# Reciprocal seed by exp of minus ln in block 0 of a fused attention, rational-FFN and gated-FFN kernel

## Chip, core and metric

One core of a Trainium2 chip. The metric is the device time of the kernel in microseconds (us). The engines are PE (TensorE, matmul), DVE (VectorE), ACT (ScalarE), POOL (GpSimd) and SP (SyncE, which issues DMAs here).

## What is computed

Three stages on 6016 tokens with 256 channels, all in 32-bit floats:

```python
qn = q / (norm(q, axis=1) + 1e-6); kn = k / (norm(k, axis=1) + 1e-6)
a = softmax(kn.T @ qn / tau)             # 256 x 256
x = v @ a                                # 6016 x 256
h = x @ w_in                             # 256 -> 2048
P = a0 + a1*h + a2*h**2 + a3*h**3
Q = 1.0 + abs(b0)*abs(h) + abs(b1)*h**2
y = (P / (Q + 1e-6)) @ w_out             # 2048 -> 256
gate = sigmoid(y @ w_gate); val = y @ w_val          # 256 -> 1536
out = (gate * val) @ w_out2              # 1536 -> 256
```

The kernel forms M = a @ w_in once, and then h = v @ M.

## The kernel before

**Tiling.** Channels lie on partitions, and the tokens are cut into 16 blocks of 376. The 2048 columns of the hidden layer are 16 tiles of 128, taken in 8 pairs. One pair of a block is a slot; a slot's tensors are 128x752 (two tiles of 376 tokens). Pairs are counted through: pair 8 is the first of block 1. Matmul operands are held as a high and a low half (hi, lo), and a product is three matmuls (`product3`, lines 721 to 723). In block 0 the second product of the rational layer is different: `add_raw_y` (L816) multiplies the undivided 32-bit values.

**A slot for pair j.** PE's `hidden` writes h to `ps_h` (12 matmuls). ACT makes `poly` = -(a3*h + a2) (L489, Identity) and `ab` = |h| (L492, Abs), then `vb` = b1*|h| + b0 (L512). DVE makes the Horner steps `poly` = poly*h (L673) and (poly - a1)*h (L684); the second one frees `ps_h` for the next `hidden`. In slot 0 poly, ab and the Horner steps are done in two halves (L483, L485, L662 to L681). Then DVE makes `quad` = vb*ab (L700), which is Q - 1. ACT makes the `seed`, an estimate of 1/Q with a sign, by reading the bits of quad as an integer and taking Sigmoid of it with a scale (L528). One slot later DVE makes t = (quad + 1)*seed (L649) in place of quad, and `scaled` = (poly - a0)*seed in place of poly (L653). ACT makes `e2` by Square of t (L467), and DVE makes the first Newton step (t - 2)*poly (`newton`, L619) and then the quotient g = (e2 + c)*poly (`quotient`, L626), which takes in a second Newton step. `g` has the same memory as `seed`. Two slots after its own, pair j's g goes into PE's product to y.

**Buffers.** `poly`, `quad` and `seed` have two buffers each, `ab`, `vb` and `e2` one. So ACT's poly waits for `g_ready` of two pairs before, and `ab` for `quad_ready` of the pair before.

**Beside it in block 0.** In slots 0 to 5 PE also makes the rest of M, tiles 4 to 11 (`M_AT`, `m_tile` L734), and ACT and DVE split them (`split_m`, L405 and L556). `hidden` waits for `m_lo_ready` of the M tiles it reads: for j = 2, 4, 6 that is one split in the slot just before. In the last slot ACT and DVE split v for block 1 (`split_v`, L399 and L550). The 13 weight chunks of the later products are split by ACT (`weights_hi`, L393) and POOL (`weights_lo`, L365): ACT takes chunk 6 + j at the end of slot j, POOL chunk 5 + j after `h_read` of slot j. SP reloads a stage when POOL is done with its last chunk, and after all of them loads v for block 1. ACT's tables: Sqrt for the norms (L421), Exp for the softmax (L435, a preload), Sigmoid from slot 0 on (L515).

**Order.** Each engine's program is written out by hand and runs in order; the engines meet at semaphores. Block 0 and block 1 are straight code, blocks 2 to 15 a loop. From block 1 on, the gated layer of the block before runs between the pairs (`gate_and_value`, `add_o`), and it begins in block 1's slot 1, after y is split (L462, L631).

Of the kernel before, what the change touches and what calls it, by code (L numbers as in the profile page):

```python
# [17 lines left out]
P = 128  # L18


def attention_rational_gated_kernel(nc, q, k, v, tau, w_in, w_out1, coef_a, coef_b, w_gate, w_val, w_out2, out):
# [58 lines left out]
    with ExitStack() as ctx:  # L80
# [40 lines left out]
        def region(at, shape):  # L121
# [12 lines left out]
        e2 = region(8 * PW, (2, TB))  # L134
        v_in = region(9 * PW, (CC, TB))
# [24 lines left out]
        consts = sb("consts", [P, 6])  # L160
        c_seed, c_square = consts[:, 0:1], consts[:, 1:2]
        norm_guard, sum_guard = consts[:, 4:5], consts[:, 5:6]

# [31 lines left out]
            sem("horner1"), sem("horner2"), sem("quad_ready"), sem("seed_ready"))  # L195
        t_ready, scaled, newton1, e2_ready, g_ready = (
# [26 lines left out]
        for n in reversed(range(T2 // 4)):  # L223
            chunks.append((w2_v[:, 4 * n:4 * n + 4, :], w2_hi[:, 4 * n:4 * n + 4, :], w2_lo[:, 4 * n:4 * n + 4, :]))
        def staged(n):
            a = chunks[n][1].shape[1]
            return stage[STAGE_OF[n]].rearrange("p (a b) -> p a b", a=a)
# [117 lines left out]
        @block.gpsimd  # L345
        def _(pool):

            nc.gpsimd.memset(consts[:, 0:1], SEED_BIAS).then_inc(o_stored, 16)
            nc.gpsimd.memset(consts[:, 1:2], -RIPPLE_D)
            nc.gpsimd.memset(consts[:, 2:3], 0.0).then_inc(g_hi_ready, PAIRS)  # L350
            nc.gpsimd.memset(consts[:, 3:4], 0.0).then_inc(g_lo_ready, PAIRS)
            nc.gpsimd.memset(norm_guard, 1e-6)
            nc.gpsimd.memset(sum_guard, 1e-9)
# [13 lines left out]

            pool.wait_ge(v_lo_ready, 1)
            for n in range(EARLY_LO):
                weights_lo(n)  # L370

            def step(i, first, carry, head, tail):
                for j, now, late, old, gone, early, second, left in slots(i, first, carry, head, tail):
                    if isinstance(i, int) and i * PAIRS + j < len(chunks) - EARLY_LO:
                        pool.wait_ge(h_read, now + 1)
                        weights_lo(EARLY_LO + now)
                    if old is not None and not unsplit(old):
                        n = j % 2
                        pool.wait_ge(g_hi_ready, old + 1)
                        wait_count(pool, y_added, old + (-1))  # L380
                        nc.gpsimd.tensor_tensor(g_lo[n], g[n], as_f32(g_hi[n]),  # L381
                                                ALU.subtract).then_inc(g_lo_ready, 1)

            steps(pool, step)


        @block.scalar
        def _(act):
# [46 lines left out]
            nc.scalar.activation(consts[:, 3:4], consts[:, 1:2], ACT.Exp)  # L435
# [32 lines left out]

            def step(i, first, carry, head, tail):
                if splits_v(i, first):  # L470
                    split_v(i)
                for j, now, late, old, gone, early, second, left in slots(i, first, carry, head, tail):
                    n, o = j % 2, (j - 1) % 2
# [6 lines left out]
                    if is_block(i, 0) and j == 0:  # L480
                        for x, done, read in ((0, h_half, h_half_read), (1, h_done, h_read)):
                            act.wait_ge(done, 1)
                            nc.scalar.activation(poly[n][:, x, :], ps_h[:, x, :], ACT.Identity, scale=neg_a[:, 3:4],  # L483
                                                 bias=neg_a[:, 2:3])
                            nc.scalar.activation(ab[:, x, :], ps_h[:, x, :], ACT.Abs).then_inc(read, 1)  # L485
                    elif now is not None:
# [6 lines left out]
                    for n_m in M_AT[j] if is_block(i, 0) and j < len(M_AT) else ():  # L493
                        split_m(n_m)
                    if is_block(i, 0) and j == PAIRS - 1:
                        split_v(1)
# [17 lines left out]
                    if is_block(i, 0) and j == 0:  # L514
# [3 lines left out]
                    if (j > 0 or not tail) and late is not None:  # L518
                        square(o, late)
                    if early is not None:  # L520
                        split_gated(*early)
                    if now is not None:
                        act.wait_ge(quad_ready, now + 1)
                        if unsplit(now) or (is_block(i, 1) and j < 2):
                            wait_count(act, y_added, now + (-1))
# [14 lines left out]
                    if isinstance(i, int) and i * PAIRS + j < len(chunks) - EARLY_HI:  # L540
                        weights_hi(EARLY_HI + now)
# [5 lines left out]
        def _(dve):  # L547
# [90 lines left out]

            def step(i, first, carry, head, tail):
                if splits_v(i, first):  # L640
                    split_v(i)
                for j, now, late, old, gone, early, second, left in slots(i, first, carry, head, tail):
                    n, o = j % 2, (j - 1) % 2
                    if j == 0 and early is not None:
                        times_value(*early)
                    if late is not None:
# [13 lines left out]
                    if is_block(i, 0) and j == 0:  # L660
                        dve.wait_ge(h_half_read, 1)
                        nc.vector.tensor_tensor(poly[n][:, 0, :], poly[n][:, 0, :], ps_h[:, 0, :],  # L662
                                                ALU.mult).then_inc(half_horner1, 1)
                        dve.wait_ge(half_horner1, 1)
                        nc.vector.scalar_tensor_tensor(out=poly[n][:, 0, :], in0=poly[n][:, 0, :], scalar=neg_a[:, 1:2],
                                                       in1=ps_h[:, 0, :], op0=ALU.add, op1=ALU.mult)
                        dve.wait_ge(h_read, 1)
                        nc.vector.tensor_tensor(poly[n][:, 1, :], poly[n][:, 1, :], ps_h[:, 1, :],
                                                ALU.mult).then_inc(horner1, 1)
                    elif now is not None:  # L670
# [6 lines left out]
                    if is_block(i, 0) and j == 0:  # L677
                        dve.wait_ge(horner1, 1)
                        nc.vector.scalar_tensor_tensor(out=poly[n][:, 1, :], in0=poly[n][:, 1, :], scalar=neg_a[:, 1:2],
                                                       in1=ps_h[:, 1, :], op0=ALU.add,  # L680
                                                       op1=ALU.mult).then_inc(horner2, 1)  # L681
                    elif now is not None:
# [7 lines left out]
                    for n_m in M_AT[j] if is_block(i, 0) and j < len(M_AT) else ():  # L690
                        split_m(n_m)
                    if is_block(i, 0) and j == PAIRS - 1:
                        split_v(1)
# [7 lines left out]
                    if (j > 0 or not tail) and late is not None:  # L701
# [206 lines left out]
```

## Time and profile before

| what | value |
|---|---|
| median of 3 runs | 1222.3 us (1221.54 to 1222.46) |
| the profiled execution | 1222.51 us, span 1220.6 us |
| mean granted TensorE clock | 0.995 |
| PE busy | 1196.8 us (98%), 6770 matmuls |
| weight loads busy (PEld) | 1168.6 us (96%) |
| DVE busy | 1074.8 us (88%), 1379 instructions |
| ACT busy | 882.7 us (72%), 1267 instructions |
| POOL busy | 250.3 us (21%), 146 instructions |
| DMA | 33.81 MB, nearly all in the first 60 us |

The chain of work that ended last is 91% PE, 5% DVE, 2% ACT. Block 0's `hidden` products start at 53.19 (pair 0), 58.77, 68.18, 76.33, 83.98, 90.41, 98.34 and 104.76 us (pair 7), block 1's first two at 112.92 and 120.40 us. All times in rows are us from the span's start; an instruction's duration can overlap the next one's by about 0.1 us on ACT and DVE, so what counts in a sum is the distance from start to start.

### The profile page before, as it was taken

The numbers are of one execution on the slowest core, as the hardware profiler recorded it, in microseconds if no ns is written. First come the engines' busy times: TensorE is split into PE (matmuls) and PEld (weight loads), VectorE is DVE, ScalarE is ACT, GpSimd is POOL, SyncE is SP. The second block draws the span as 40 slices with busy tenths as digits, with TensorE's granted clock in tenths as the row PEclk, the third lists the DMA queues.
The fourth block names the chain that finished last, engine by engine and source line by source line (L and its number), as shares of the span: only waits on it lengthen the run. The fifth ranks groups of instructions, "written<-read, shape, count | busy, mean of one in ns | idle before, by whom it ended". The sixth has DMA issues, their size and how long they took to land.

```text
span 1220.6 us, 19533 instructions
## 1 busy us (share of the span) xinstructions
PE 1196.8 (98%) x6770; PEld 1168.6 (96%) x6770; DVE 1074.8 (88%) x1379; ACT 882.7 (72%) x1267; POOL 250.3 (21%) x146
## 2 busy tenths in 40 slices
PE   9977899999999999999999999999999999999998
PEld 8855799999999999999999999999999999999998
DVE  7689999998998999999898989989899999989843
ACT  6877778777786777778686777777677677868632
POOL 0432112211221221212121212122122121212110
PEclk9989999999999999999999999999999999999999
DMA  9810000000000000000000000000000000000000
GB/s 368 291 65 13 2 13 1 14 13 13 13 13 13 13 0 13 13 13 13 13 13 9 4 13 13 13 13 13 13 6 7 13 13 13 13 0 13 0 14 13
DMA packets 15866, 33.81 MB, mean 28 GB/s; under 512 B 1382, under 2 KB 6246, under 8 KB 15846
## 3 DMA queue, kind: packets, MB, share of 16 engines
q1 hardware_dynamic: 14982, 32.51, 7.5%
q10 hardware_dynamic: 864, 1.05, 0.3%
q8 instruction: 11, 0.18, 0.1%
q14 instruction: 9, 0.07, 0.0%
HBM read 27.39 MB, written 6.16 MB: 27 GB/s over the span
## 4 chain that ended last, share of the span: by engine, by line
PE 91%; DVE 5%; ACT 2%; issue 2%; DMA 0%; DVEq 0%; ACTq 0%
PE ps L721 17%; PE ps L723 17%; PE ps L722 17%; PE ps L804 7%; PE ps L805 7%; PE ps L806 6%; PE ps L838 5%; PE ps L840 5%; PE ps L839 5%; PE ps L763 4%; DVE work L673 1%; DVE work L700 1%; DVE work L619 1%; ACT work L489 1%; ACT work L492 1%
## 5 line engine op out<-in xcount | busy, mean ns | idle before, releaser
L381 POOL TENSOR_TENSOR g_parts<-work,g_parts 128x752 fp32r<-128x752 f32 x120 | 218.7, 1822 | 838.5 <-ACT g_parts L503 838.5
L489 ACT ACTIVATE work<-ps,neg_a 128x752 f32<-128x752 f32 x127 | 124.5, 981 | 149.8 <-PE ps L723 87.8
L721 PE MATMUL ps<-v_hi,m_hi 128*128 128x376 f32 x512 | 173.4, 339 | 14.2 <-DVE m_lo L556 7.7
L723 PE MATMUL ps<-v_hi,m_lo 128*128 128x376 f32 x512 | 172.8, 337 | 0.0
L722 PE MATMUL ps<-v_lo,m_hi 128*128 128x376 f32 x512 | 171.7, 335 | 0.0
L804 PE MATMUL ps<-g_parts,w_hi 128*128 128x376 f32 x480 | 160.5, 334 | 0.0
L805 PE MATMUL ps<-g_parts,w_hi 128*128 128x376 f32 x480 | 160.0, 333 | 0.0
L806 PE MATMUL ps<-g_parts,w_lo 128*128 128x376 f32 x480 | 159.4, 332 | 0.0
L673 DVE TENSOR_TENSOR work<-work,ps 128x752 f32<-128x752 f32 x127 | 118.5, 933 | 42.1 <-ACT work L492 40.3
L528 ACT ACTIVATE work<-work,consts 128x752 f32<-128x752 int32 x128 | 117.6, 919 | 51.9 <-DVE work L700 51.9
L614 DVE TENSOR_TENSOR work<-work,ps 128x376 f32<-128x376 f32 x192 | 103.6, 540 | 52.3 <-PE ps L723 39.4
L467 ACT ACTIVATE work<-work,consts 128x752 f32<-128x752 f32 x128 | 118.0, 922 | 24.7 <-DVE work L649 24.7
L626 DVE SCALAR_TENSOR_TENSOR work<-work 128x752 f32<-128x752 f32 x128 | 122.1, 954 | 14.2
L456 ACT ACTIVATE ys<-work 128x376 fp32r<-128x376 f32 x192 | 98.6, 514 | 45.0 <-PE ps L840 44.9
L721 PE MATMUL ps<-ys,wg_hi 128*128 128x376 f32 x384 | 128.0, 333 | 3.2 <-DVE ys L631 2.7
L512 ACT ACTIVATE work<-work,abs_b 128x752 f32<-128x752 f32 x128 | 130.4, 1019 | 0.2
L838 PE MATMUL ps<-ys,w_hi 128*128 128x376 f32 x384 | 129.1, 336 | 0.2 <-DVE ys L636 0.2
L684 DVE SCALAR_TENSOR_TENSOR work<-work,neg_a,ps 128x752 f32<-128x752 f32 x127 | 126.3, 995 | 3.0
L723 PE MATMUL ps<-ys,wv_lo 128*128 128x376 f32 x384 | 128.7, 335 | 0.0
L700 DVE TENSOR_TENSOR work<-work 128x752 f32<-128x752 f32 x128 | 128.5, 1004 | 0.1
L723 PE MATMUL ps<-ys,wg_lo 128*128 128x376 f32 x384 | 128.5, 335 | 0.0
L840 PE MATMUL ps<-ys,w_lo 128*128 128x376 f32 x384 | 128.5, 335 | 0.0
(113 smaller groups left out, 2846.3 us busy)
## 6 DMA issues: line engine op xcount, KB each, us to landing
work<-in_v SPq DMA_DIRECT2D x16, 376.0 KB, 3.0
out<-work SPq DMA_DIRECT2D x15, 376.0 KB, 2.3
kq<-in_k SPq DMA_DIRECT2D x9, 512.0 KB, 12.9
kq<-in_q SPq DMA_DIRECT2D x9, 512.0 KB, 15.1
before<-in_moe_w_out SPq DMA_DIRECT2D x5, 512.0 KB, 12.6
before<-in_moe_w_in SPq DMA_DIRECT2D x8, 256.0 KB, 7.3
before<-in_moe_w_gate SPq DMA_DIRECT2D x2, 512.0 KB, 9.5
before<-in_moe_w_val SPq DMA_DIRECT2D x2, 512.0 KB, 6.7
```

Source lines behind the costliest of these rows:

```text
L381: nc.gpsimd.tensor_tensor(g_lo[n], g[n], as_f32(g_hi[n]), ALU.subtract).then_inc(g_lo_ready, 1)
L489: nc.scalar.activation(poly[n], ps_h, ACT.Identity, scale=neg_a[:, 3:4], bias=neg_a[:, 2:3])
L673: nc.vector.tensor_tensor(poly[n], poly[n], ps_h, ALU.mult).then_inc(horner1, 1)
L700: nc.vector.tensor_tensor(quad[n], vb, ab, ALU.mult).then_inc(quad_ready, 1)
L721: nc.tensor.matmul(dst, l_hi, r_hi, start=(n == 0), stop=False)
L722: nc.tensor.matmul(dst, l_hi, r_lo, start=False, stop=False)
L723: last = nc.tensor.matmul(dst, l_lo, r_hi, start=False, stop=(n == len(parts) - 1))
L804: nc.tensor.matmul(acc_y[:, c, :], l_hi, r_hi, start=(j == 0 and x == 0), stop=False)
L805: nc.tensor.matmul(acc_y[:, c, :], l_hi, r_lo, start=False, stop=False)
L806: last = nc.tensor.matmul(acc_y[:, c, :], l_lo, r_hi, start=False, stop=(j == PAIRS - 1 and x == 1))
L838: nc.tensor.matmul(acc_o[:, c, :], l_hi, s_hi[n], start=(m == 0), stop=False)
L840: last = nc.tensor.matmul(acc_o[:, c, :], l_lo, s_hi[n], start=False, stop=(m == T2 - 1))
```

## The change

In block 0 alone, the seed is made as exp(-ln(quad + 1 + 1e-6)) by two ScalarE activations (Ln with the bias `q_one`, then Exp with scale -1), instead of the integer Sigmoid. The seed is positive now. The Square and the first Newton step are gone; the quotient is (t - 2)*poly. The region of `e2` serves as a third `poly` buffer (`first_poly`), so poly of pair j waits for the quotient of pair j - 3. The slot's instructions have an order of their own (`first_slot`): on ACT poly, ab, up to two M splits, v split, vb, a third M split, then the seed of pair j - 1 (in slot 0: of pair 0; in slot 1: none), then the weight copy; on DVE the Horner steps, the M splits, quad of pair j, then t and scaled of pair j - 1 (again pair 0 in slot 0, none in slot 1), and the quotient of pair j - 1. Pair 7's seed, t, scaled and quotient stand in block 1's slot 0, and the load of the Sigmoid table behind its Exp. The preload before the softmax is an Ln instead of an Exp. ACT's and POOL's weight chunks move one slot later from slot 1 on. `newton1` and `e2_ready` are raised by 8 at the start, since block 0 no longer counts them.

```diff
+        first_poly = poly + [e2]
...
+            nc.gpsimd.memset(q_one, Q_ONE)
...
-                    if isinstance(i, int) and i * PAIRS + j < len(chunks) - EARLY_LO:
+                    if is_block(i, 0) and j != 1 or is_block(i, 1) and j == 0:
                         pool.wait_ge(h_read, now + 1)
-                        weights_lo(EARLY_LO + now)
+                        weights_lo(EARLY_LO + max(now - 1, 0))
...
-            nc.scalar.activation(consts[:, 3:4], consts[:, 1:2], ACT.Exp)
+            nc.scalar.activation(consts[:, 3:4], consts[:, 0:1], ACT.Ln)
...
+            def first_seed(pair):
+
+                act.wait_ge(quad_ready, pair + 1)
+                wait_count(act, y_added, pair - 1)
+                nc.scalar.activation(seed[pair % 2], quad[pair % 2], ACT.Ln, bias=q_one).then_inc(logs, 1)
+                act.wait_ge(logs, pair + 1)
+                nc.scalar.activation(seed[pair % 2], seed[pair % 2], ACT.Exp, scale=-1.0).then_inc(seed_ready, 1)
...
+                    act.wait_ge(h_done, j + 1)
+                    wait_count(act, g_ready, j - 2)
+                    nc.scalar.activation(p, ps_h, ACT.Identity, scale=neg_a[:, 3:4], bias=neg_a[:, 2:3])
+                    act.wait_ge(quad_ready, j)
+                    nc.scalar.activation(ab, ps_h, ACT.Abs).then_inc(h_read, 1)
...
+                if j != 1:
+                    first_seed(max(j - 1, 0))
+                if j > 0:
+                    weights_hi(EARLY_HI + j - 1)
...
-                    if is_block(i, 0) and j == 0:
+                    if is_block(i, 1) and j == 0:
+                        first_seed(PAIRS - 1)
                         nc.scalar.activation(consts[:, 2:3], consts[:, 1:2], ACT.Sigmoid)
...
+            def first_seeded(pair):
+
+                n, p = pair % 2, first_poly[pair % 3]
+                dve.wait_ge(seed_ready, pair + 1)
+                nc.vector.scalar_tensor_tensor(out=quad[n], in0=quad[n], scalar=Q_ONE, in1=seed[n],
+                                               op0=ALU.add, op1=ALU.mult).then_inc(t_ready, 1)
+                dve.wait_ge(horner2, pair + 1)
+                nc.vector.scalar_tensor_tensor(out=p, in0=p, scalar=neg_a[:, 0:1], in1=seed[n],
+                                               op0=ALU.add, op1=ALU.mult).then_inc(scaled, 1)
+
+            def first_quotient(pair):
+
+                dve.wait_ge(t_ready, pair + 1)
+                dve.wait_ge(scaled, pair + 1)
+                nc.vector.scalar_tensor_tensor(out=g[pair % 2], in0=quad[pair % 2], scalar=-2.0,
+                                               in1=first_poly[pair % 3], op0=ALU.add,
+                                               op1=ALU.mult).then_inc(g_ready, 1)
...
+                first_quad(j)
+                for n_m in tiles[2:]:
+                    split_m(n_m)
+                if j != 1:
+                    first_seeded(max(j - 1, 0))
+                if j > 0:
+                    first_quotient(j - 1)
```

## Rows read from the trace of the kernel before

**Rows 1.** Stretches: window, then each engine's busy us, PE clock, DMA share.
```profile
80.00:90.00 10.00, 9.09 (x33) 5.72 (x32) 9.76 (x12) 8.65 (x12) 3.95 (x2) 1.00 0.28 93
...
180.00:190.00 10.00, 10.00 (x60) 10.00 (x59) 8.89 (x11) 5.92 (x8) 1.82 (x1) 1.00 0.12 39
```

**Rows 2.** Waits of PE, whole span: us in total, times, longest us.
```profile
PE ps L721 <- DVE m_lo L556: 7.7, 3, 5.4
...
PE ps L721 <- DVE v_lo L550: 2.2, 1, 2.2
```

**Rows 3.** Timeline of DVE, slot 4: start us, us, instruction, [idle before <- releaser].
```profile
88.38 0.94 DVE L673 TENSOR_TENSOR work<-work,ps 128x752 f32<-128x752 f32 x1
89.35 1.00 DVE L684 SCALAR_TENSOR_TENSOR work<-work,neg_a,ps 128x752 f32<-128x752 f32 x1
90.27 0.75 DVE L556 SCALAR_TENSOR_TENSOR m_lo<-ps,small,m_hi 128x512 fp32r<-128x512 f32 x1
90.93 0.93 DVE L700 TENSOR_TENSOR work<-work 128x752 f32<-128x752 f32 x1
91.78 0.94 DVE L619 SCALAR_TENSOR_TENSOR work<-work 128x752 f32<-128x752 f32 x1
92.82 0.94 DVE L626 SCALAR_TENSOR_TENSOR work<-work 128x752 f32<-128x752 f32 x1
93.68 0.93 DVE L649 SCALAR_TENSOR_TENSOR work<-work 128x752 f32<-128x752 f32 x1
94.53 0.99 DVE L653 SCALAR_TENSOR_TENSOR work<-work,neg_a 128x752 f32<-128x752 f32 x1
```

**Rows 4.** Timeline of ACT, slot 4.
```profile
86.68 0.98 ACT L489 ACTIVATE work<-ps,neg_a 128x752 f32<-128x752 f32 x1
87.56 0.79 ACT L492 ACTIVATE work<-ps 128x752 f32<-128x752 f32 x1
...
88.81 1.02 ACT L512 ACTIVATE work<-work,abs_b 128x752 f32<-128x752 f32 x1
...
91.89 0.93 ACT L528 ACTIVATE work<-work,consts 128x752 f32<-128x752 int32 x1 [1.26 <-DVE work L700]
```

**Rows 5.** Timeline of PE, slot 4: first hidden matmul, M tile, raw y, next hidden.
```profile
83.98 0.41 PE L721 MATMUL ps<-v_hi,m_hi 128*128 128x376 f32 x1 [0.91 <-DVE m_lo L556]
...
86.11 1.88 PE L734 MATMUL ps<-before 128*128 128x512 f32 x4
87.83 2.69 PE L816 MATMUL ps<-work,before 128*128 128x376 f32 x8
90.41 0.44 PE L721 MATMUL ps<-v_hi,m_hi 128*128 128x376 f32 x1
```

**Rows 6.** Timeline of ACT, slot 0: vb, table load, seed.
```profile
59.55 1.00 ACT L512 ACTIVATE work<-work,abs_b 128x752 f32<-128x752 f32 x1
60.57 1.28 ACT L515 ACT_TABLE_LOAD   x1
...
61.97 0.91 ACT L528 ACTIVATE work<-work,consts 128x752 f32<-128x752 int32 x1
```

**Rows 7.** Timeline of PE, slot 2: first hidden matmul and M tile.
```profile
68.18 0.65 PE L721 MATMUL ps<-v_hi,m_hi 128*128 128x376 f32 x1 [5.39 <-DVE m_lo L556]
...
72.08 2.17 PE L734 MATMUL ps<-before 128*128 128x512 f32 x4
```

**Rows 8.** A stretch in the gap before slot 2, columns as in rows 1.
```profile
66.00:68.00 2.00, 0.00 (x0) 0.00 (x0) 1.97 (x4) 1.66 (x2) 1.81 (x1) 0.50 0.00 0
```

**Rows 9.** Timeline of POOL and of DVE, slot 6.
```profile
102.78 2.37 POOL L365 TENSOR_TENSOR w_lo<-work,w_hi 128x1024 fp32r<-128x1024 f32 x1 [4.81 <-ACT work L492]
...
104.62 1.33 DVE L700 TENSOR_TENSOR work<-work 128x752 f32<-128x752 f32 x1
```

**Rows 10.** Timeline, block 1: t of pair 8 on DVE, first gate product on PE.
```profile
122.92 0.93 DVE L649 SCALAR_TENSOR_TENSOR work<-work 128x752 f32<-128x752 f32 x1
...
127.72 0.44 PE L721 MATMUL ps<-ys,wg_hi 128*128 128x376 f32 x1 [1.86 <-DVE ys L631]
```

More of the change, by code:

```diff
@@ L351, in _ @@
             nc.gpsimd.memset(consts[:, 3:4], 0.0).then_inc(g_lo_ready, PAIRS)
-            nc.gpsimd.memset(norm_guard, 1e-6)
-            nc.gpsimd.memset(sum_guard, 1e-9)
+            nc.gpsimd.memset(norm_guard, 1e-6).then_inc(newton1, PAIRS)
+            nc.gpsimd.memset(sum_guard, 1e-9).then_inc(e2_ready, PAIRS)
+            nc.gpsimd.memset(q_one, Q_ONE)
             nc.gpsimd.memset(ones[:], 1.0).then_inc(consts_ready, 1)
@@ L467, in square, with first_slot @@
                 nc.scalar.activation(e2, quad[o], ACT.Square, scale=RIPPLE_D, bias=c_square).then_inc(e2_ready, 1)
+            def first_seed(pair):
[4 more added lines that the diff above has]
+                nc.scalar.activation(seed[pair % 2], seed[pair % 2], ACT.Exp, scale=-1.0).then_inc(seed_ready, 1)
+            def first_slot(j):
+                p = first_poly[j % 3]
+                if j == 0:
+                    for x, done, read in ((0, h_half, h_half_read), (1, h_done, h_read)):
+                        act.wait_ge(done, 1)
+                        nc.scalar.activation(p[:, x, :], ps_h[:, x, :], ACT.Identity, scale=neg_a[:, 3:4],
+                                             bias=neg_a[:, 2:3])
+                        nc.scalar.activation(ab[:, x, :], ps_h[:, x, :], ACT.Abs).then_inc(read, 1)
+                else:
+                    act.wait_ge(h_done, j + 1)
[3 more added lines that the diff above has]
+                    nc.scalar.activation(ab, ps_h, ACT.Abs).then_inc(h_read, 1)
+                tiles = M_AT[j] if j < len(M_AT) else ()
+                for n_m in tiles[:2]:
+                    split_m(n_m)
+                if j == PAIRS - 1:
+                    split_v(1)
+                act.wait_ge(h_read, j + 1)
+                nc.scalar.activation(vb, ab, ACT.Identity, scale=abs_b[:, 1:2],
+                                     bias=abs_b[:, 0:1]).then_inc(vb_ready, 1)
+                for n_m in tiles[2:]:
+                    split_m(n_m)
+                if j != 1:
+                    first_seed(max(j - 1, 0))
+                if j > 0:
+                    weights_hi(EARLY_HI + j - 1)
             def step(i, first, carry, head, tail):
@@ L479, in step @@
                         square(o, late)
-                    if is_block(i, 0) and j == 0:
[L481 to L486, printed above, removed]
+                    if now is not None:
                         act.wait_ge(h_done, now + 1)
@@ L517, in step @@
                         split_y(i)
-                    if (j > 0 or not tail) and late is not None:
+                    if (j > 0 or not tail) and late is not None and not unsplit(late):
                         square(o, late)
@@ L523, in step @@
                         act.wait_ge(quad_ready, now + 1)
-                        if unsplit(now) or (is_block(i, 1) and j < 2):
-                            wait_count(act, y_added, now + (-1))
+                        if is_block(i, 1) and j < 2:
+                            act.wait_ge(y_added, now - 1)
                         else:
@@ L637, in split_gated, with first_quad @@
                                         ALU.subtract).then_inc(s_lo_ready, 1)
+            def first_quad(pair):
+                dve.wait_ge(vb_ready, pair + 1)
+                nc.vector.tensor_tensor(quad[pair % 2], vb, ab, ALU.mult).then_inc(quad_ready, 1)
+            def first_seeded(pair):
[6 more added lines that the diff above has]
+                                               op0=ALU.add, op1=ALU.mult).then_inc(scaled, 1)
@@ L645, in step @@
                         times_value(*early)
-                    if late is not None:
+                    if late is not None and not unsplit(late):
                         dve.wait_ge(seed_ready, late + 1)
@@ L659, in step @@
                         quotient(o, late)
[L660 to L670, printed above, removed]
+                    if now is not None:
                         dve.wait_ge(h_read, now + 1)
@@ L676, in step @@
                         times_value(*early)
[L677 to L682, printed above, removed]
+                    if now is not None:
                         dve.wait_ge(horner1, now + 1)
@@ L689, in step @@
                         split_gated(*left)
[L690 to L693, printed above, removed]
                     if j == y_split_at(i) and head:
@@ L700, in step @@
                         nc.vector.tensor_tensor(quad[n], vb, ab, ALU.mult).then_inc(quad_ready, 1)
-                    if (j > 0 or not tail) and late is not None:
+                    if late is not None and unsplit(late):
+                        first_seeded(late)
+                        first_quotient(late)
+                    elif (j > 0 or not tail) and late is not None:
                         newton(o, late)
```

44 lines of the change are left out of this document (36 added, 8 removed).

## Prediction

> **What bounds the kernel now.** I read the page first, then the busy time by stretches, then who waits for whom on PE, then the stretch of block 0 instruction by instruction on each engine. Over the whole span PE is near its full share, and from about 170 us on it has no gap: a stretch such as 180 to 190 us is 10.00 us of matmul [rows 1]. There nothing that VectorE or ScalarE save can move the end. Block 0 and the head of block 1, about 55 to 128 us, are different: in 80 to 90 us VectorE is busy for 9.76 us of 10 and PE for 9.09 [rows 1]. PE's waits are nearly all in this region, and the largest are for VectorE results: 7.7 us for the low half of M, 2.2 for the low half of v [rows 2]. So the end is set by PE, but PE's work behind 128 us starts as late as block 0 lets it, and a microsecond won there is won at the end, as long as the state in which block 1 begins is the same.
>
> I call one pass over a pair of FF tiles a slot; its landmarks are hidden(j) on PE, then Identity and Abs on ScalarE (poly, ab), then the two Horner steps on VectorE, which release hidden(j+1). VectorE's slot 4 has eight instructions: Horner 1 at 88.38, Horner 2 at 89.35, M split 90.27, quad 90.93, first Newton 91.78, quotient 92.82, t 93.68, scaled 94.53, whose end at 95.52 the next Horner follows at once: a period of some 7.2 us [rows 3]. The last step carries a small wait: Horner 1 starts 0.03 us after ab ends (87.56 + 0.79 = 88.35), and ab follows poly, which starts at 86.68, just behind the quotient two pairs back [rows 4]. PE needs 2.13 us for hidden, 1.72 for the M tile and 2.58 for the raw y product, together 6.43 [rows 5]. VectorE is therefore what is full, with a buffer wait (poly is written only after the old quotient) beside it.
>
> **The change, part by part.** (1) Newton removed. In block 0 one VectorE instruction of a pitch of 1.04 us (91.78 to 92.82) goes from each slot [rows 3]. What is left is 0.97 + 0.92 + 0.66 + 0.85 + 0.86 (t) + 1.09 (scaled, whose result the quotient now waits for: 0.99 busy and a handover of 0.1 like the one from Newton to quotient) + 0.86 = 6.21 us. (2) ScalarE: Square and Sigmoid become Ln and Exp, of the same 128x752 shape. No row has Ln or an Exp of that shape. The bounds are the cheapest row of this size that reads PSUM, 0.79, and the dearest, 1.02 with two pointer operands [rows 4]; I take 0.93, that of the seed's Sigmoid at 91.89, the nearest in form. Exp waits for Ln itself, another 0.1; behind it on ScalarE stand the weight copy and the next poly, which PE's hidden product releases later anyway. ScalarE's slot works 7.2 less the 1.26 us in which it waits for quad [rows 4] = 5.9 us, and with two instructions swapped for two of the same size it stays at 6.0, below VectorE's 6.2, with seeds ready at about the moment quad ends; 0.1 us more on each would be 0.1 to 0.2 a slot on the path. (3) The third poly buffer takes away the wait of poly for the quotient. What is late next is the loop through PE. Where hidden(j+1) also needs an M split (j = 1, 3, 5): hidden 2.29 to its end (its last matmul, 0.33 long, starts 0.17 before the M tile's first), 0.88 + 0.79 for poly and ab, 0.97 + 0.92 + 0.75 on VectorE, 0.2 of handovers: 6.8 us. Where it doesn't, PE's own 6.43. (4) The weight copies and their POOL halves shift one slot down. They move data needed first in block 1: POOL's last one starts in block 1's first slot, lasts 2.37 [rows 9], and PE's second slot there waits for it; by the sum below it is ready at 114.1, while the raw y behind it waits until 117.7. Free; uncovered it would cost some 0.5 us. SP's reloads of the stages wait for those POOL halves and so also start a slot later; each has two more slots before its copy. One extra memset on POOL ahead of the ones: 0.03 us, ahead of a DMA-bound stretch. Nothing.
>
> (5) Slots 0 and 1. Before, vb(0), the table load of 1.28 us and the seed stand between slot 0 and poly(1) [rows 6], and VectorE has to take t and scaled first; M split(7) comes late, and hidden(2) starts at 68.18 [rows 7]. After: quad(0) right behind the two M splits, 58.66 to 59.85 (0.94 plus 0.25 for an overlap with POOL, see below), M split(6) in between, Ln 59.9, Exp 60.87 to 61.75, no load, poly(1) 61.66, ab to 63.33, t and scaled until 63.6, Horner 63.56 and 64.53, M split 65.45 to 66.2, hidden(2) 66.34: 1.84 us earlier.
> (6) From there at PE's high clock: hidden(3) 72.8 (+6.43), (4) 79.6 (+6.8), (5) 86.0, (6) 92.8, with no M tile (7) 99.0 (the raw y product waits for the quotient, then 2.58), and (8) 106.3: 2.3 for hidden, 1.7 for ab, 0.97 + 0.92, then v's low half, 1.24 from start to start as for a quad beside POOL. VectorE on POOL's heels pays: quad takes 1.33 instead of 0.94 us when 0.5 us of it lie beside POOL [rows 9]; that is in slots 6 to 8, as before.
> (7) Slot 8 is bound otherwise: poly(8) uses the old two buffers and waits for quotient(6), which ends at 103.01 + 0.97 + 0.92 + 1.24 + 0.85 + 0.86 + 1.09 + 0.94 = 109.9. Then 0.1 + 1.7 to Horner 1, and 0.97 + 0.92 + 1.25 + 0.86 + 1.09 + 0.86 = 5.95: t(8) at 117.6, where it was at 122.92 [rows 10]. ScalarE in that slot has Ln, Exp, the moved table load and the Sigmoid: done at about 116.8, 0.8 us early. From t(8) on the code is the same, so PE's gate product comes at 127.72 - 5.3 = 122.4 [rows 10], and with it the end.
> The Trainium skill, ScalarE: Activation LUTs, section "What ACT_TABLE_LOAD costs", says a switch costs a drain of about 1.38 us besides the 1.28. The rows disagree: the load begins right behind the vb before it and the seed's Sigmoid starts at 61.97, 1.40 us after the load's start. By the page the moved load would be 0.5 us too late in slot 8, and the sum 4.0 instead of 4.5.
>
> (8) The clock. PE stood still before hidden(2) for 5.39 us, in that gap the granted clock fell to 0.50 (1.2 GHz) [rows 8], and from hidden's start to the M tile's it took 72.08 - 68.18 = 3.90 us, against 86.11 - 83.98 = 2.13 at the high level, 2.4 GHz [rows 5, 7]: 1.8 more. The new gap runs from 62.8 to 66.3, 3.5 us. The next longest gap, the 2.2 us of v's low half [rows 2], lies in block 1's first slot. So a fall is likely, for part of the product; I take 0.8 of the 1.8, with 0 and 1.8 as ends. Behind it the loops are tight and hand a delay on whole. Sum: 5.3 - 0.8 = 4.5 us.
>
> The profiled execution took 1222.5 us (span 1220.6), the median of the three runs is 1222.3: no difference that matters. 1222.5 - 4.5 = 1218.0, and from the median 1217.8, which I give.
>
> **The rivals.** *A, the forecast*: gain 3 to 6 us, 1216.3 to 1219.3, by the ends of the clock and 0.1 us a slot on Ln and Exp. Chance 0.70. Inside it, without a fall of the clock, 1217.0.
> *B, ScalarE becomes the bound.* The seed is placed after vb, though its quad was ready a slot earlier. If Ln and Exp together take 0.8 us more than 1.9 (both beyond the dearest row), t waits 0.7 us in six slots: 4.2 of the 4.5 go, 1222.0. Against it: all ScalarE rows of 752 columns lie in 0.79 to 1.02. Chance 0.12, spread between 1220 and 1222.5.
> *C, the clock stays low* over two or three slots because PE's share is still small: another 1.5 us, 1219.4. For it: PE's low share in slots 6 and 7. Chance 0.09.
> *D, slower: Ln and Exp don't share a table.* Then each seed costs ScalarE two loads of 1.29 us [rows 6]: 5.9 + 2.6 = 8.5 us a slot against the present 7.2, 1.3 in each of seven slots, and about 1 more in the softmax: 1222.5 + 10 = 1232.6. It decides from the point where loads take more than 7.2 - 5.9 = 1.3 us a slot, so one load would nearly do. The trace has one load each for the Sqrt, Exp and Sigmoid stages, and none with Ln. For me against it: the change's own preload is an Ln, with only Exp behind. Chance 0.09. The same skill page, section "Table sets: the hidden batching unit", lists a set that holds exp and ln, one load for both; by it D is out, and no row of this trace can show it.
> That the change doesn't do what it says would be D, or a Newton left in; the diff leaves none in block 0.
>
> **How the numbers follow.** The likeliest is A, 1217.8. A and C are faster by over 0.2% (2.4 us, about what a measurement of this kernel can tell from no change), 0.79; B is within 0.2% for most of it, 0.12; D is slower, 0.09. The range takes A whole with a little below for a cheaper Ln, C, and half of B: 1215.8 to 1221.0; D and the rest of B are left out.
>
> **What would show each step.** Four table loads in all, the last in block 1's first slot. Ln and Exp at 0.85 to 1.0 us. VectorE's slot at 6.4 to 6.8 us instead of 7.2, alternating. hidden(2) near 66.3, hidden(8) near 106.3 (or up to 1.8 later), the first gate product near 122 to 123. ab(j) no longer behind the quotient. The prediction is wrong if VectorE waits for ScalarE's Exp before t in most slots, if loads appear between Ln and Exp, or if PE's gaps behind 128 us grow by what was won.

## The result

| | before | after |
|---|---|---|
| median | 1221.9 us (4 runs, 1221.05 to 1222.46) | 1236.7 us (4 runs, 1235.53 to 1238.74) |
| profiled execution | 1222.5 us, span 1220.6 | 1238.7 us, span 1236.8 |
| DVE busy | 1074.8 us | 1068.5 us |
| ACT busy | 882.7 us | 904.7 us |
| ACT_TABLE_LOAD | 4 | 21 |

The changed kernel is slower by 1.2%: ratio 1.0123, 95% interval 1.0106 to 1.0141. The forecast of 1217.8 us with a range up to 1221.0 was wrong, in sign too. What came true is rival D, to which the prediction gave 9 in 100.

The groups of ScalarE's instructions by line show it at once (line, engine, operation, count, busy us and mean ns of one, idle before):

```profile
L479 ACT ACT_TABLE_LOAD x8 | 10.3, 1283 | 0.1
L481 ACT ACT_TABLE_LOAD x8 | 10.3, 1283 | 0.1
...
L479 ACT ACTIVATE work<-work,consts 128x752 f32<-128x752 f32 x8 | 7.4, 924 | 0.1
...
L481 ACT ACTIVATE work<-work 128x752 f32<-128x752 f32 x8 | 6.7, 832 | 0.1
...
L445 ACT ACT_TABLE_LOAD x1 | 1.3, 1283 | 0.0
```

L479 is Ln and L481 Exp. Each of the eight has a table load of its own, 16 loads or 20.6 us, and L445 is one more in the softmax: with the preload turned into an Ln, the softmax's Exp finds the wrong set. Ln and Exp themselves cost 0.92 and 0.83 us, inside the bounds set.

The timeline of ScalarE through one slot (pair 4), where rows 4 stood before:

```profile
90.64 0.98 ACT L495 ACTIVATE work<-ps,neg_a 128x752 f32<-128x752 f32 x1 [0.27 <-PE ps L800]
91.52 0.79 ACT L497 ACTIVATE work<-ps 128x752 f32<-128x752 f32 x1
92.36 0.69 ACT L411 ACTIVATE m_hi<-ps,small 128x512 fp32r<-128x512 f32 x1
92.95 1.00 ACT L504 ACTIVATE work<-work,abs_b 128x752 f32<-128x752 f32 x1
93.97 1.28 ACT L479 ACT_TABLE_LOAD   x1
95.26 0.93 ACT L479 ACTIVATE work<-work,consts 128x752 f32<-128x752 f32 x1
96.20 1.28 ACT L481 ACT_TABLE_LOAD   x1
97.50 0.83 ACT L481 ACTIVATE work<-work 128x752 f32<-128x752 f32 x1
98.23 1.04 ACT L399 ACTIVATE wv_hi<-before 128x1024 fp32r<-128x1024 f32 x1
99.18 0.96 ACT L495 ACTIVATE work<-ps,neg_a 128x752 f32<-128x752 f32 x1
```

From poly to poly is 8.54 us, 2.57 of it loads, and ScalarE waits for nothing between them (the 0.27 us shown lie ahead of the first poly): it has become the full engine. VectorE, which set the pace before [rows 3], now waits 1.7 to 3.6 us for each Exp. The longest waits of VectorE and PE in 40 to 200 us (us in total, times, longest):

```profile
DVE work L683 <- ACT work L481: 19.9, 8, 3.6
...
PE ps L893 <- DVE work L693: 15.9, 6, 3.6
...
PE ps L798 <- DVE m_lo L592: 5.8, 1, 5.8
```

Where the time comes from along the way: poly(4) starts at 90.64 instead of 86.68, poly(7) at 115.85 instead of 107.95, poly(8) at 126.53 instead of 116.58, and the first gate product on PE at 143.87, where it was at 127.72 [rows 10]. That is 10 us by block 1's first slot and 6.2 more in the next two; behind the gate product nothing is left to lose, and the span is 16.2 us longer. PE's timeline of this last stretch:

```profile
126.49 2.79 PE L893 MATMUL ps<-work,before 128*128 128x376 f32 x8 [1.96 <-DVE work L693]
...
130.69 0.44 PE L798 MATMUL ps<-v_hi,m_hi 128*128 128x376 f32 x1 [1.40 <-POOL w_lo L371]
...
136.63 5.38 PE L893 MATMUL ps<-work,before 128*128 128x376 f32 x8 [3.62 <-DVE work L693]
...
143.87 0.44 PE L798 MATMUL ps<-ys,wg_hi 128*128 128x376 f32 x1 [1.86 <-DVE ys L667]
```

The raw y product of pair 7 waits 3.62 us for a quotient with its two loads, and then takes 5.38 us instead of 2.79, because behind that gap the granted clock is at the lower level, 1.2 GHz (0.50 in the stretches from 136 to 142 us, 1.00 from 130 to 134).

### The profile page after: what moved, and what is told of

The parts are those of the page before. It is cut to its first block, busy times and chain, and to the rows that moved or that the text cites. A ratio compares the mean times of both kernels' runs of the same rounds, so it can differ in the third digit from the quotient of the medians.

```text
span 1236.8 us, 19529 instructions
## 1 busy us (share of the span) xinstructions
PE 1203.0 (97%) x6770; PEld 1170.4 (95%) x6770; DVE 1068.5 (86%) x1371; ACT 904.7 (73%) x1284; POOL 250.8 (20%) x147
## 4 chain that ended last, share of the span: by engine, by line
PE 88%; ACT 4%; DVE 4%; issue 2%; DMA 1%; SPq 1%; DVEq 0%; ACTq 0%
PE ps L800 17%; PE ps L798 17%; PE ps L799 17%; PE ps L881 6%; PE ps L882 6%; PE ps L883 6%; PE ps L915 5%; PE ps L917 5%; PE ps L916 5%; DMA kq<-in_q 1%; PE ps L893 1%; PE ps L811 1%; SPq L308 1%; ACT L479 1%; SPq L310 1%
## 5 line engine op out<-in xcount | busy, mean ns | idle before, releaser
L530 ACT ACTIVATE work<-ps,neg_a 128x752 f32<-128x752 f32 x120 | 117.8, 982 | 147.6 <-PE ps L800 84.3
L756 DVE TENSOR_TENSOR work<-work,ps 128x752 f32<-128x752 f32 x120 | 112.0, 933 | 40.9 <-ACT work L533 39.1
L566 ACT ACTIVATE work<-work,consts 128x752 f32<-128x752 int32 x120 | 110.2, 918 | 41.7 <-DVE work L774 41.7
L798 PE MATMUL ps<-ys,wg_hi 128*128 128x376 f32 x384 | 128.0, 333 | 3.2 <-DVE ys L667 2.7
L915 PE MATMUL ps<-ys,w_hi 128*128 128x376 f32 x384 | 129.2, 336 | 0.2 <-DVE ys L672 0.2
L473 ACT ACTIVATE work<-work,consts 128x752 f32<-128x752 f32 x120 | 110.7, 922 | 24.7 <-DVE work L742 24.7
L799 PE MATMUL ps<-ys,wg_hi 128*128 128x376 f32 x384 | 127.9, 333 | 0.0
L916 PE MATMUL ps<-ys,w_hi 128*128 128x376 f32 x384 | 127.9, 333 | 0.0
L799 PE MATMUL ps<-ys,wv_hi 128*128 128x376 f32 x384 | 127.8, 333 | 0.0
L798 PE MATMUL ps<-ys,wv_hi 128*128 128x376 f32 x384 | 127.6, 332 | 0.0
```

What stands on the lines that cost most here:

```text
L798: nc.tensor.matmul(dst, l_hi, r_hi, start=(n == 0), stop=False)
L799: nc.tensor.matmul(dst, l_hi, r_lo, start=False, stop=False)
L915: nc.tensor.matmul(acc_o[:, c, :], l_hi, s_hi[n], start=(m == 0), stop=False)
L916: nc.tensor.matmul(acc_o[:, c, :], l_hi, s_lo[n], start=False, stop=False)
```

## The experiments

Theory 1: the table loads are the whole loss, and without them the prediction's sum holds. Theory 2: the new order, the chain of Ln and Exp and PE's clock lose as well. Ratios are to the kernel before on the same chip; a difference in us between two kernels that ran on different chips can hold the few tenths by which the medians of the kernel before differ (1221.9 to 1222.3).

**One table set.** The changed kernel with the set named that holds both functions:

```diff
+            nc.scalar.preload_act_table_set("natural_log_exp_and_others")
             nc.scalar.activation(consts[:, 3:4], consts[:, 0:1], ACT.Ln)
```

> The changed kernel with one line more: the table set that holds both ln and exp is named and loaded at the Ln preload, so that the 16 loads around the eight seeds and the extra one in the softmax go. Theory 1 (the loads are the whole loss, and the sum of the prediction holds otherwise): 1217.8 us, 1216 to 1219.5. Theory 2 (the new order, the Ln to Exp chain and PE's low clock lose as well): between 1222 and 1230.

Measured: 1219.0 us (1217.84 to 1219.70), ratio 0.9975 (0.9965 to 0.9986). One line is worth 17.7 us, and turns a loss of 1.2% into a gain of 0.25%. Four loads are left in all. The timeline of VectorE in slot 4 and the next Horner step:

```profile
82.79 0.94 DVE L713 TENSOR_TENSOR work<-work,ps 128x752 f32<-128x752 f32 x1 [0.51 <-ACT work L498]
...
86.19 0.93 DVE L684 SCALAR_TENSOR_TENSOR work<-work 128x752 f32<-128x752 f32 x1
87.04 0.99 DVE L687 SCALAR_TENSOR_TENSOR work<-work,neg_a 128x752 f32<-128x752 f32 x1
88.15 0.94 DVE L694 SCALAR_TENSOR_TENSOR work<-work 128x752 f32<-128x752 f32 x1
89.09 0.94 DVE L713 TENSOR_TENSOR work<-work,ps 128x752 f32<-128x752 f32 x1
```

From Horner to Horner is 6.30 us here and 6.80 in the slots with the small wait at their end, in turn, where the prediction had 6.43 and 6.8. t (L684) no longer waits for Exp.

**The same once more**, beside the kernels further below.

> The kernel with one table set once more, beside the one with throwaway matmuls on the same chip: 1219.0, 1218.4 to 1219.6.

Measured: 1219.4 us (1217.90 to 1220.02), ratio 0.9975 (0.9965 to 0.9986).

**One load a seed.** The same kernel with one load of that set before each Ln, that is half of the changed kernel's loads around the seeds:

```diff
+                nc.scalar.preload_act_table_set("natural_log_exp_and_others")
                 nc.scalar.activation(seed[pair % 2], quad[pair % 2], ACT.Ln, bias=q_one).then_inc(logs, 1)
```

> The kernel with one table set, and one load of that same set before each Ln: half of the loads of the changed kernel. Theory 1 with loads paid in full on ScalarE's path: halfway between the one with none and the changed kernel, about 1227. Rival (a slot of 7.2 us has room for one load, 5.9 + 1.3 = 7.2): at most 2 to 3 us above the one with none, about 1220.

Measured: 1228.1 us (1226.91 to 1228.62), ratio 1.0050 (1.0035 to 1.0066). With 0, 8 and 16 loads around the seeds the times are 1219.0, 1228.1 and 1236.7: 9.1 us for the first eight, 8.6 for the rest, about 1.1 us for each load of 1.28. There is no room for even one, although ScalarE has idle time of 0.4 to 0.9 us a slot without loads: a load sits between vb and Exp, in the chain on which t and the quotient wait.

**Loads in the kernel before.**

```diff
                         act.wait_ge(quad_ready, now + 1)
...
+                        if is_block(i, 0):
+                            nc.scalar.preload_act_table_set("exp_and_others")
+                            nc.scalar.preload_act_table_set("sigmoid_and_others")
                         nc.scalar.activation(seed[n], quad[n].bitcast(I32), ACT.Sigmoid, scale=SEED_SCALE,
```

> The kernel before, with two table loads ahead of each seed of block 0 and nothing else changed. Theory 1: ScalarE's slot goes from 5.9 to 8.5 us against 7.2, so about 8 x 1.3 to 8 x 2.6 more: 1232 to 1243. Theory 2: the loads hide in ScalarE's wait of 1.26 us for quad and cost under 8 us: below 1230.

Measured: 1238.3 us (1237.99 to 1238.71), ratio 1.0133 (1.0118 to 1.0149). 16 loads alone, put into the kernel before, cost 16.3 us, as much as the whole loss of the changed kernel and more. They stand behind the wait for quad, so this kernel doesn't show what loads would cost that could hide in it. Theory 2 falls for the sign; what it says of the size comes with the clock, below.

**The last seed without loads.** The changed kernel, with the common set loaded at the end of slot 7, where ScalarE waits anyway:

```diff
                 if j > 0:
                     weights_hi(EARLY_HI + j - 1)
+                if j == PAIRS - 1:
+                    nc.scalar.preload_act_table_set("natural_log_exp_and_others")
```

> The changed kernel, but the set with ln and exp is loaded once ScalarE has done slot 7's work and waits, so that the seed of pair 7, the last of block 0, has no load in its chain; the 14 loads of the other seven seeds stay. Theory (behind the last pair nothing overlaps, PE stands still for it and its clock falls, so its two loads cost more than the average 2.2 us a pair): 3 to 5.5 us faster than the changed kernel, 1231.2 to 1233.7. Rival (each load costs the same wherever it stands, about 1.1 us): 1234.5.

Measured: 1232.7 us (1231.67 to 1233.26), ratio 1.0083 (1.0068 to 1.0099): 4.0 us faster than the changed kernel for two loads of 1.28 us, nearly twice the average of 2.2 us a pair. PE's timeline has the reason. The wait for pair 7's quotient is down from 3.62 to 1.21 us, and the product is at the high clock:

```profile
132.95 2.79 PE L895 MATMUL ps<-work,before 128*128 128x376 f32 x8 [1.21 <-DVE work L695]
...
137.60 0.44 PE L800 MATMUL ps<-ys,wg_hi 128*128 128x376 f32 x1 [1.86 <-DVE ys L669]
```

**Two poly buffers.** The kernel with one table set, with the third buffer undone (the indices too):

```diff
-        first_poly = poly + [e2]
+        first_poly = poly
...
-                    wait_count(act, g_ready, j - 2)
+                    wait_count(act, g_ready, j - 1)
```

> The kernel with one table set, but two poly buffers in block 0 instead of three. Theory (the third buffer frees poly from the quotient): poly waits for the quotient of pair j - 2 again, which stands at the end of the slot before; 0.3 to 0.7 us in each of six slots, so 2 to 4 us more than with three. Rival: the loop through PE hides it, within 1 us.

Measured: 1226.0 us (1224.17 to 1227.30), ratio 1.0031 (1.0022 to 1.0040): 7.0 us more than with three, where 2 to 4 were expected, and slower than the kernel before. VectorE's timeline:

```profile
92.94 0.94 DVE L694 SCALAR_TENSOR_TENSOR work<-work 128x752 f32<-128x752 f32 x1
95.67 0.94 DVE L713 TENSOR_TENSOR work<-work,ps 128x752 f32<-128x752 f32 x1 [1.79 <-ACT work L498]
```

In the new order the quotient (L694) is the last instruction of a slot. With two buffers poly can start only behind it, and VectorE stands still for 1.79 us while ScalarE makes poly and ab. The third buffer is no small addition to the change: the order doesn't work without it.

**One more VectorE instruction.** The kernel with one table set, with an instruction of the Newton step's size in front of the quotient:

```diff
+                nc.vector.scalar_tensor_tensor(out=first_poly[pair % 3], in0=quad[pair % 2], scalar=0.0,
+                                               in1=first_poly[pair % 3], op0=ALU.add,
+                                               op1=ALU.mult).then_inc(stepped, 1)
+                dve.wait_ge(stepped, pair + 1)
```

> The kernel with one table set, and one more VectorE instruction of the Newton step's size, in its place, for each of the eight pairs of block 0 (the factor t where the removed step had t - 2, so the output carries a little more error). Theory (VectorE's slot of 6.2 us is close to PE's loop of 6.4 to 6.8, so the removal was worth about 0.5 us a slot and a full 1.0 us twice at the end): 1219.0 + 5 = 1224, between 1222.5 and 1226. Rival (PE and ScalarE bound the slots without it): within 1.5 us of 1219.0.

Measured: 1226.9 us (1225.27 to 1228.61), ratio 1.0039 (1.0023 to 1.0054): 7.9 us, or 1.0 us for each of the eight, and above the range that was expected (up to 1226). The slot goes to 7.2 us (Horner at 78.58, 85.77 and 92.95). In part the price is the clock again: PE's raw y product takes 2.79 us in slot 5, but 4.36 and 4.49 in slot 6 and in block 1's first, behind waits of 2.3 us:

```profile
93.09 2.79 PE L898 MATMUL ps<-work,before 128*128 128x376 f32 x8 [0.62 <-DVE work L698]
...
100.28 4.36 PE L898 MATMUL ps<-work,before 128*128 128x376 f32 x8 [2.26 <-DVE work L698]
...
116.33 4.49 PE L898 MATMUL ps<-work,before 128*128 128x376 f32 x8 [2.31 <-DVE work L698]
```

**Newton's step left out, nothing else.** The kernel before, in which the eight pairs of block 0 skip `newton` (its counter is raised by 8 at the start instead). The quotient of block 0 then lacks its factor t - 2 and is wrong; only the time of this kernel is of use.

```diff
                 dve.wait_ge(scaled, pair + 1)
+                if unsplit(pair):
+                    return
                 nc.vector.scalar_tensor_tensor(out=poly[o], in0=quad[o], scalar=-2.0, in1=poly[o],
```

> The kernel before with the first Newton step left out for the eight pairs of block 0 and nothing else changed; the division there is less exact. Theory (a VectorE instruction of 1.04 us a slot is worth what lies between VectorE's 7.2 us and PE's loops of 6.4 to 6.8): 3 to 6 us faster, 1216.5 to 1219.5. Rival (without the third poly buffer and the new order, poly's wait for the quotient and the table load in slot 0 keep the slots at over 6.8): 0.5 to 2.5 us faster.

Measured: 1221.5 us (1219.60 to 1222.22), ratio 0.9990 (0.9980 to 0.9999), 0.8 us. The rival's number is right, and of its reasons the table load in slot 0: hidden(2) starts at 68.28 us, as before. In the later slots it is something that neither named. ScalarE's timeline and VectorE's:

```profile
86.38 0.96 ACT L489 ACTIVATE work<-ps,neg_a 128x752 f32<-128x752 f32 x1
...
89.41 0.91 ACT L467 ACTIVATE work<-work,consts 128x752 f32<-128x752 f32 x1
91.57 0.93 ACT L528 ACTIVATE work<-work,consts 128x752 f32<-128x752 int32 x1 [1.26 <-DVE work L702]
92.40 1.04 ACT L393 ACTIVATE w_hi<-before 128x1024 fp32r<-128x1024 f32 x1
93.34 0.96 ACT L489 ACTIVATE work<-ps,neg_a 128x752 f32<-128x752 f32 x1
...
95.02 0.94 DVE L675 TENSOR_TENSOR work<-work,ps 128x752 f32<-128x752 f32 x1 [0.64 <-ACT work L492]
...
97.57 0.94 DVE L702 TENSOR_TENSOR work<-work 128x752 f32<-128x752 f32 x1
```

Poly follows the weight copy without a wait, and ScalarE's only gap is the 1.26 us in which the seed waits for quad of its own slot. So a loop is closed over both engines: seed, copy, poly and ab on ScalarE, then two Horner steps, the M split and quad on VectorE, then the next seed. It takes 6.96 us, against 7.2 before: it was hardly less bound than VectorE's own work. The profile is of one of the faster executions: its first gate product comes 2.7 us earlier than before, and four of the ten runs are at 1219.6 to 1220.3 us with a mean granted clock of 0.997; the other six are at 1221.5 to 1222.2 with 0.994 to 0.996. PE's waits have grown with the shorter slots (3.05 us ahead of pair 8), and a lower clock goes with the slower six, so part of what the step gives is probably lost there; no profile of one of the six was taken. The changed kernel also moves the seed behind the quad of the pair after, and that wait is gone from its timeline. The Newton step alone is worth little; with the moved seed and the third buffer the slot goes from 7.2 to 6.3 and 6.8 us. The moved seed by itself was not tried.

**PE's clock.** The profile of the kernel with one table set has its first gate product at 121.44 us, 6.3 us earlier than before [rows 10], but its span is only 4.6 us shorter. The stretches tell why (window, busy us of PE, PEld, DVE, ACT, POOL, then the granted clock):

```profile
120.00:122.00 2.00, 0.56 (x3) 0.56 (x4) 2.00 (x3) 1.22 (x2) 0.00 (x0) 1.00 0.00 0
122.00:124.00 2.00, 2.00 (x9) 2.00 (x8) 1.89 (x3) 1.36 (x2) 0.00 (x0) 0.54 0.03 8
124.00:126.00 2.00, 2.00 (x9) 2.00 (x8) 1.04 (x3) 0.00 (x0) 0.00 (x0) 0.61 0.00 0
```

PE's timeline there, and the last row again from the kernel before:

```profile
108.97 2.79 PE L894 MATMUL ps<-work,before 128*128 128x376 f32 x8 [1.35 <-DVE work L694]
...
113.16 0.44 PE L799 MATMUL ps<-v_hi,m_hi 128*128 128x376 f32 x1 [1.40 <-POOL w_lo L371]
...
116.78 2.79 PE L894 MATMUL ps<-work,before 128*128 128x376 f32 x8 [1.30 <-DVE work L694]
...
121.44 0.44 PE L799 MATMUL ps<-ys,wg_hi 128*128 128x376 f32 x1 [1.86 <-DVE ys L668]
...
131.13 0.44 PE L799 MATMUL ps<-v_hi,m_hi 128*128 128x376 f32 x1 [1.71 <-DVE work L763]
...
135.85 0.44 PE L721 MATMUL ps<-v_hi,m_hi 128*128 128x376 f32 x1 [1.71 <-DVE work L684]
```

Behind PE's gap ahead of the gate product the clock falls to 1.2 GHz for some 3 us, which costs 1.6 us: from the gate product to the next product that waits for VectorE it takes 131.13 - 121.44 = 9.69 us, and 135.85 - 127.72 = 8.13 in the kernel before. The second profile of the same kernel has the fall there too (9.70 us), and another at pair 2 (clock 0.60 in 66 to 70 us); its span is 2.2 us longer, 0.7 of it because pair 2 starts later. The first profile has a mean clock of 0.999, the second 0.997; of the 16 runs of this kernel the five with 0.999 took 1217.8 to 1218.8 us and the eleven with 0.997 took 1218.7 to 1220.0. So throwaway matmuls were put into PE's gaps, into PSUM banks that are free there:

```diff
+            def keep_warm(count, bank):
+                for _ in range(count):
+                    nc.tensor.matmul(ps[:, bank, 0:P], ones[:], ones[:], start=True, stop=True)
...
+                        keep_warm(4, 2)
                         pe.wait_ge(w_lo_ready, len(chunks))
...
+                    if is_block(i, 0) and j == 1:
+                        keep_warm(12, 0)
                     if old is not None and unsplit(old):
+                        if old >= 4:
+                            keep_warm(4, 2)
                         add_raw_y(old)
+                        if old == PAIRS - 1:
+                            keep_warm(6, 2)
```

A first kernel had twice as many of them (24, 8, 8 and 10):

> The kernel with one table set, and throwaway 128-column matmuls of ones into PSUM banks that are free, in PE's gaps of block 0 and block 1's first slots (24 ahead of pair 2's hidden product, 8 or 10 in each of the later gaps), so that PE's granted clock doesn't fall. Theory (the clock's fall, in one place or another, takes 1.5 to 2 us of the gain, which is why the kernel with one table set gave 2.9 and not 5 to 6): 1216.0 to 1217.3, and a narrower spread than 1217.8 to 1219.7. Rival (the missing part goes to something else, such as PE's gaps behind 128 us): 1218.5 to 1219.5, and later than that if the throwaway matmuls delay the real ones.

Measured: 1218.9 us (1218.55 to 1219.36), ratio 0.9972 (0.9961 to 0.9983). This is the rival's number, not the theory's 1216.0 to 1217.3. The clock is at 1.00 throughout and the spread narrower, but the time is the same, since 24 of them outlast the gap:

```profile
61.94 5.52 PE L831 MATMUL ps<-ones 128*128 128x128 f32 x48
```

They keep PE until 67.5 us, where pair 2's product had started at 65.65. The later groups of 8 take 1.95 us each, in gaps of 1.3 to 1.7. With half of them:

> As the kernel with one table set and throwaway matmuls, but half as many: a call of it took 0.24 us and not the 0.12 reckoned with, so that 24 ran 5.5 us in a gap of 3.4 and pushed pair 2's hidden product back by 1.8. Now 12 there (2.9 us), 4 in the gaps of 1.3 to 1.7 (1.0 us) and 6 ahead of the first gate product (1.5 us of 1.9). Theory (the clock's fall takes 1.5 to 2 us): 1216.0 to 1217.5. Rival (PE's clock costs nothing in the median): 1218.5 to 1219.5.

Measured: 1215.9 us (1215.75 to 1216.83), ratio 0.9947 (0.9934 to 0.9961), the fastest of all, 0.1 us below what the theory gave, and 3.5 us under the kernel with one table set beside it (1219.4). Two falls of 1.4 and 1.6 us, which most runs of that kernel have by their mean clock, make 3.0 of the 3.5; the rest is not explained. PE's timeline at the same place, with 0.72 us of the gap left over:

```profile
62.53 2.84 PE L831 MATMUL ps<-ones 128*128 128x128 f32 x24
66.09 0.41 PE L799 MATMUL ps<-v_hi,m_hi 128*128 128x376 f32 x1 [0.72 <-DVE m_lo L593]
...
119.87 1.50 PE L831 MATMUL ps<-ones 128*128 128x128 f32 x12
121.90 0.44 PE L799 MATMUL ps<-ys,wg_hi 128*128 128x376 f32 x1 [0.53 <-DVE ys L668]
...
130.03 0.44 PE L799 MATMUL ps<-v_hi,m_hi 128*128 128x376 f32 x1 [1.71 <-DVE work L763]
```

From the gate product to the next waiting one are 8.13 us again. The same two additions in the kernel before:

> The kernel before with the same throwaway matmuls. If PE's low clock costs the kernel before what its timeline shows (VectorE idle for 1.5 us in slot 2 and 0.9 us in block 1's first slot behind slow hidden products), 1.5 to 2.4 us faster: 1219.6 to 1220.5. Rival (VectorE-bound slots swallow it): 1221.5 to 1222.

Measured: 1222.9 us (1222.06 to 1223.11), ratio 1.0004 (0.9995 to 1.0013).

> The kernel before with the same halved throwaway matmuls, all of them now shorter than the gaps they stand in, but for those ahead of raw y products that hardly waited (0.4 us or none): there up to 0.9 us of delay each. Theory of the clock: 1220 to 1221.5. Rival: 1222 or more.

Measured: 1221.9 us (1220.10 to 1223.90), ratio 0.9997 (0.9988 to 1.0007). There is no gain to be told there, where the theory had 1219.6 to 1220.5 and 1220 to 1221.5. Part of the matmuls stand ahead of products that hardly waited and push these back. In the second kernel the clock also still falls in the profile, to 0.50 in 112 to 114 us, behind a wait of 2.21 us that no throwaway matmul fills. So neither shows what the clock alone costs the kernel before; that was not separated.

## Why the prediction was wrong

**The step that failed** is rival D's chance, and with it the term for table loads around Ln and Exp, which the sum has at nothing: they cost 17.7 us. The prediction saw that the trace couldn't show where a load for Ln would be put, priced it with the right mechanism (10 us of loss), and then held the diff's own preload against it ("the change's own preload is an Ln, with only Exp behind"). That is an argument from what the author of the change meant, not from a row. It should have stood as an open condition, a loss of 10 us against a gain of 4.5: at even odds between the two cases the change loses. The range left it out.

The Trainium skill, ScalarE: Activation LUTs, section "Table sets: the hidden batching unit", says that one set has exp and ln, one load for both. The set is there, as the kernel with one table set shows; but that it exists didn't mean that it was picked. The changed kernel got a load before each Ln and another before each Exp, and a single load for all eight seeds only where the code named the common set. The prediction gave this as a ground against D; the measurement decides otherwise.

**D's size.** Its slot of 8.5 us was right (8.54 between two polys), and so was its 10 us up to block 1's first slot. Its 1232.6 was 4 us short of the median, most likely for what lies behind the last pair: there is no next pair to work on, the loads are paid whole, and PE, idle for 3.6 us, does the next product at half its clock. The kernel without loads in the last seed puts that at 4.0 us.

**The sum without the loads** held in its landmarks, but not in its total: the gain forecast was 4.5 us, the one measured in the median 2.9. Row by row, in the profile of the kernel with one table set, and the value of the prediction beside it (its block 0 begins 0.5 us earlier than the kernel before's): hidden(2) 65.65 (66.3), hidden(8) 105.30 (106.3), quotient(6)'s end 108.9 (109.9), t(8) 116.65 (117.6), gate product 121.44 (122.4); profiled execution 1217.9 us (1218.0 for the trace, 1217.8 for the median). That last agreement is in part luck: 0.5 us is the earlier start of block 0, which the second profile doesn't have, another 0.4 lies in the slots, and the clock took 1.6 us where 0.8 was reckoned. It is also one of the five faster runs of 16. The first median, 1219.0, lies in the range given for A (up to 1219.3), the second, 1219.4, just beyond it.
- (1) The removal of Newton's step: as a term it was right in this order, even low: 1.0 us a pair and not what lies between 7.2 and the loop through PE. As an edit by itself it was worth 0.8 us in all.
- (2) Ln and Exp: 0.92 and 0.83 us against 0.93 taken for each. Rival B falls.
- (3) The third buffer: sized at a wait "beside" the full engine; in the new order it is worth 7.0 us. The loop through PE is 6.80 us, as said. But PE's own 6.43 in the other slots was too much: the 2.58 us for the raw y product held a wait for the Horner step, which ends at 90.35 us [rows 3, 5], and where the next product follows at once it is 69.50 to 71.74, 2.24 us. VectorE's order sets these slots, at 6.30 where the prediction had 6.21.
- (4) The moved weight halves: PE does wait 1.40 us for POOL's last one, and the raw y behind it still waits 1.30 for its quotient. Free, as said.
- (7) The moved load of the Sigmoid table: it stands at 113.41 and the next Sigmoid starts at 114.81, 1.40 us after it; no drain shows behind it. The drain of about 1.38 us that the Trainium skill, ScalarE: Activation LUTs, section "What ACT_TABLE_LOAD costs", adds for a switch is in none of these traces: in the changed kernel Ln begins at 95.26, 1.29 us after its load does.
- (8) The clock: the price of a fall was near, 1.4 us at pair 2 (3.53 us from hidden(2) to the M tile against 2.14) and 1.6 at the gate product, where 1.8 was given; their number wasn't. It came behind the gap ahead of pair 2 in one profile of two, and in both behind the one ahead of the gate product, where the shortened slots leave PE several gaps of 1.3 to 1.9 us close together. The prediction had none there. Rival C, a low clock for longer than in one slot, gave 1219.4, and the two medians are near its number. But its mechanism isn't what the profiles show: the clock doesn't stay low over slots, it falls a second time 50 us later. That the number fits is luck.

## What to carry to other kernels

Before a ScalarE function is swapped for another, ask which table set the built program will hold at that point, count the loads in the built program, and name the set when one serves both. A load in a chain on which another engine waits costs nearly its whole 1.28 us, even where ScalarE has idle time elsewhere in the slot. And price an edit with its partners: taking an instruction from the fullest engine gives little (0.8 us here for eight instructions of 1.04) while a second loop, here the one through ScalarE's order, is 0.2 us behind it.

## What the runs showed of the hardware

- A table load took 1.28 us in every kernel here, even when it was of the set that was there already: the kernel with one load a seed loads the same set over again and pays 1.1 us for each of the eight.
- PE's clock was lost behind a number of short gaps with work between them (1.35, 1.40, 1.30 and 1.86 us), not only behind a long one (5.39 us in the kernel before). In the kernel before the same gap of 1.86 us, with 1.02 and 0.39 ahead of it, left the clock up. Filling a part of each with throwaway products was enough to keep it at 2.4 GHz in the profile, and the kernel took 3.5 us less of 1219.4. One such 128-column call in 32-bit floats took 0.24 us (2.84 us for 12), as two instructions, so that a count reckoned from the 0.12 us of one instruction filled twice the time that was meant.
